# Attention output of batches two to eight from rounded parts and rests, three matmuls for one in fp32, with the units' steps moved

## The reference

```
q_s = exp(q - max_d q);  q_s = q_s / (sum_d q_s + 1e-9)
k_s = exp(k - max_s k);  k_s = k_s / (sum_s k_s + 1e-9)
kv  = k_s^T v                     (64 x 64 for each head)
attn = q_s kv                     -> x: 4608 tokens x 512
x = square(relu(x w_in)) w_out                               (512 -> 2048 -> 512)
x = rmsnorm(x) * rms_g;  out = (silu(x w_gate) * (x w_val)) w_out2   (512 -> 1536 -> 512)
```

## Time and profile before

| | us |
|---|---|
| median of 3 runs | 1733.18 |
| lowest and highest | 1731.26, 1733.26 |
| the profiled execution, whole | 1731.07 |
| its span from the first to the last instruction | 1729.3 |
| PE busy | 1697.3 (98%) |
| DVE, ACT, POOL busy | 1018.1, 567.7, 567.3 |
| mean granted TensorE clock | 0.997 |

### The profile page before, as it was taken

One profiled execution on the slowest core, in us unless ns is written; L12 is line 12 of the kernel. 1 busy time (PEld: TensorE's weight loads), 2 busy tenths in 40 slices (PEclk: granted clock), 3 DMA queues, 4 the chain that ended last, 5 costly groups with the idle time before them and its releaser, 6 DMA issues.

```text
span 1729.3 us, 23832 instructions
## 1 busy us (share of the span) xinstructions
PE 1697.3 (98%) x8954; PEld 1499.7 (87%) x8954; DVE 1018.1 (59%) x1525; ACT 567.7 (33%) x952; POOL 567.3 (33%) x442
## 2 busy tenths in 40 slices
PE   6999999999999999999999999999999999999999
PEld 5989999999988888888889898888899998888887
DVE  6667576667575778788776466446554455222220
ACT  5444333333232333333334333323333334212220
POOL 2554233323202224342255745546445521000000
PEclk9999999999999999999999999999999999999999
DMA  7575455445283353334342222242222245343341
GB/s 236 193 213 168 147 167 173 161 152 183 84 265 98 122 163 120 116 121 126 118 127 95 95 97 102 76 143 80 99 99 77 77 152 181 122 146 122 122 134 49
DMA packets 136722, 230.10 MB, mean 133 GB/s; under 512 B 12192, under 2 KB 59808, under 8 KB 136608
## 3 DMA queue, kind: packets, MB, share of 16 engines
q1 hardware_dynamic: 136608, 228.57, 40.6%
HBM read 143.59 MB, written 84.93 MB: 132 GB/s over the span
## 4 chain that ended last, share of the span: by engine, by line
PE 88%; DVE 5%; POOL 3%; issue 1%; ACT 1%; DMA 1%; SPq 0%; ACTq 0%; POOLq 0%; DVEq 0%
PE bank L1590 15%; PE bank L1592 14%; PE bank L1591 14%; PE bank L1676 7%; PE bank L1678 7%; PE bank L1677 7%; PE bank L1747 6%; PE bank L1748 6%; PE bank L1746 6%; PE bank L1564 2%; PE bank L1583 1%; DVE TAR L1296 1%; PE bank L1579 1%; POOL ssq L869 1%; DMA W<-in_w 0%
## 5 line engine op out<-in xcount | busy, mean ns | idle before, releaser
L1590 PE MATMUL bank<-TR,SW 128*128 128x460 f32 (+1 forms) x840 | 310.8, 370 | 2.2 <-ACT group L1142 1.8
L1591 PE MATMUL bank<-TR,SW 128*128 128x460 f32 (+1 forms) x840 | 310.1, 369 | 0.0
L1592 PE MATMUL bank<-TR,SW 128*128 128x460 f32 (+1 forms) x840 | 310.1, 369 | 0.0
L1590 PE MATMUL bank<-TAR,SA 128*128 128x288 f32 x784 | 247.8, 316 | 3.9 <-DVE TAR L1296 2.4
L1591 PE MATMUL bank<-TAR,SA 128*128 128x288 f32 x784 | 231.8, 296 | 0.0
L1592 PE MATMUL bank<-TAR,SA 128*128 128x288 f32 x784 | 231.2, 295 | 0.0
L1676 PE MATMUL bank<-GH,W 128*128 128x512 f32 x576 | 224.3, 389 | 0.7 <-DVE GH L1316 0.7
L1678 PE MATMUL bank<-GH,W 128*128 128x512 f32 x576 | 224.1, 389 | 0.0
L1677 PE MATMUL bank<-GH,W 128*128 128x512 f32 x576 | 224.1, 389 | 0.0
L1590 PEld LDWEIGHTS bank<-TR,SW 128*128 128x128 f32 x840 | 158.0, 188 | 21.9 <-issue 3.1
L1592 PEld LDWEIGHTS bank<-TR,SW 128*128 128x128 f32 x840 | 158.1, 188 | 16.7
(11 more groups left out here) (144 smaller groups left out, 2817.5 us busy)
## 6 DMA issues: line engine op xcount, KB each, us to landing
h_scratch<-hb SPq DMA_DIRECT2D x128, 288.0 KB, 2.7
hst<-h_scratch SPq DMA_DIRECT2D x144, 256.0 KB, 2.7
AR<-a_scratch SPq DMA_DIRECT2D x54, 512.0 KB, 3.7
a_scratch<-group SPq DMA_DIRECT2D x96, 230.0 KB, 2.0
xst<-xn_scratch SPq DMA_DIRECT2D x16, 920.0 KB, 5.0
xn_scratch<-x SPq DMA_DIRECT2D x9, 1024.0 KB, 5.3
out<-ost SPq DMA_DIRECT2D x36, 256.0 KB, 4.5
kt<-in_k SPq DMA_DIRECT2D x28, 320.0 KB, 4.5
```

Of the source, the lines that this page charges most:

```text
L1590: nc.tensor.matmul(ps[:, 0:w], w_hi[:, cc], x_hi[:, c], start=opens and c == 0, stop=False, skip_group_check=True)
L1591: nc.tensor.matmul(ps[:, 0:w], w_lo[:, cc], x_hi[:, c], start=False, stop=False, skip_group_check=True)
L1592: last = nc.tensor.matmul(ps[:, 0:w], w_hi[:, cc], x_lo[:, c], start=False, stop=c == 1, skip_group_check=True)
```

## The change

X0 and X1 of batches 1 to 7 become three fp32r matmuls. readQ0 and readQ1 on ACT now write the rounded part of qT (`qT` has two planes); two new DVE tasks `restQ0` and `restQ1` subtract that from the PSUM bank into the second plane. KV is read into `bd32`; a new ACT task `highKV` copies it, rounded, to `bdhi`, and a new DVE task `restKV` makes `bdlo`. A round that takes the bank of a Q round also waits for its rest (`q_rest`); X0 and X1 wait for `kv_rest` and `q_rest`. The tables move: the base of a unit is one step earlier, X0, X1 and their reads stay where they were, KM and KV come one step earlier, Q0 and Q1 with their reads two steps earlier, qmax, qsub, qexp, qsum, qinv and qnorm two steps earlier. A memory address (`STAT_END`) is fixed.

```diff
-UNIT_BASE = [[8 + 12 * c for c in range(KC)]] + [[6 + 11 * c for c in range(KC)]] * (B - 2)
-UNIT_PE = [("KM", -4), ("Q0", 0), ("Q1", 1), ("KV", 2), ("X0", 6), ("X1", 7)]
-UNIT_DVE = [("qmax", -10), ("qsum", -6), ("qinv", -6), ("kmax", -9), ("readKM", -3), ("readKV", 3)]
-UNIT_ACT = [("qexp", -7), ("kexp", -2), ("readQ0", 1), ("readQ1", 2), ("readX0", 7), ("readX1", 8)]
-UNIT_POOL = [("qsub", -9), ("qnorm", -4)]
+UNIT_BASE = [[7 + 12 * c for c in range(KC)]] + [[5 + 11 * c for c in range(KC)]] * (B - 2)
+UNIT_PE = [("KM", -4), ("Q0", -1), ("Q1", 0), ("KV", 2), ("X0", 7), ("X1", 8)]
+UNIT_DVE = [("qmax", -11), ("qsum", -7), ("qinv", -7), ("kmax", -9), ("readKM", -3), ("restQ0", 1), ("restQ1", 2),
+            ("readKV", 3), ("restKV", 5)]
+UNIT_ACT = [("qexp", -8), ("kexp", -2), ("readQ0", 0), ("readQ1", 1), ("highKV", 4), ("readX0", 8), ("readX1", 9)]
+UNIT_POOL = [("qsub", -10), ("qnorm", -5)]
 UNIT_SP = [("q", -20), ("kT", -19), ("kt", -17), ("v", -15)]
...
+        def rest_no(b, c, half):
+            return 2 * (unit(b, c) - KC - 1) + half + 1
...
                 wait_taken(eng, n - 2)
+                b, kind, c = ROUNDS[n - 2]
+                if kind[0] == "Q":
+                    eng.wait_ge(q_rest, rest_no(b, c, int(kind[1])))
...
+            def kv_hi(b, c):
+
+                wait_taken(act, ROUND_NO[b, "KV", c] - 1)
+                nc.scalar.activation(bdhi[:, :], bd32[:, :], ACT.Copy).then_inc(kv_high, 1)
...
+            def q_lo(b, c, half):
+
+                n = ROUND_NO[b, f"Q{half}", c]
+                cols = slice(0, Q_CUT * P) if half == 0 else slice(Q_CUT * P, S)
+                wait_taken(dve, n - 1)
+                nc.vector.tensor_tensor(qT[:, 1, cols], round_bank(n - 1)[:, 0:cols.stop - cols.start], f(qT[:, 0, cols]),
+                                        ALU.subtract).then_inc(q_rest, 1)
+
+            def kv_lo(b, c):
+
+                dve.wait_ge(kv_high, unit(b, c) - KC)
+                nc.vector.tensor_tensor(bdlo[:, :], bd32[:, :], f(bdhi[:, :]), ALU.subtract).then_inc(kv_rest, 1)
...
+                elif b:
+                    tok = slice(half * TA, (half + 1) * TA)
+                    pe.wait_ge(kv_rest, u - KC)
+                    pe.wait_ge(q_rest, rest_no(b, c, half))
+                    nc.tensor.matmul(ps[:, 0:TA], bdhi[:, :], qT[:, 0, tok], start=True, stop=False)
+                    nc.tensor.matmul(ps[:, 0:TA], bdlo[:, :], qT[:, 0, tok], start=False, stop=False)
+                    last = nc.tensor.matmul(ps[:, 0:TA], bdhi[:, :], qT[:, 1, tok], start=False, stop=True)
```

More of the change, by code:

```diff
@@ L25 @@
 NB4 = TB // P
+STAT_END = 211744
 EPS_RMS, EPS_SUM = 1e-6, 1e-9
@@ L300, in build @@
         ssqlo, at = place("ssqlo", at, [P, TB], F32R)
-        stat_end = at
+        assert at <= STAT_END
+        stat_end = at = STAT_END
         ones, at = place("ones", at, [P, P], F32R)
@@ L336, in build @@
         vn[1], at = place("vn1", at, [P, SJ, P + 1])
+        bd32, at = place("bd32", at, [P, P])
         assert at <= quad_at
@@ L342, in build @@
             kt[i], at = place(f"kt{i}", at, [P, SJ, P])
-        qT, at = place("qT", at, [P, S])
-        bd, at = place("bd", at, [P, P])
+        qT, at = place("qT", at, [P, 2, S], F32R)
+        bdlo, at = place("bdlo", at, [P, P], F32R)
+        bdhi, at = place("bdhi", at, [P, P], F32R)
         kmax, at = place("kmax", at, [P, 1])
@@ L386, in build @@
         q_sum, q_den, q_inv, q_norm = sem("q_sum"), sem("q_den"), sem("q_inv"), sem("q_norm")
+        q_rest, kv_high, kv_rest = sem("q_rest"), sem("kv_high"), sem("kv_rest")
         rnd_ready, taken_act, taken_dve = sem("rnd_ready"), sem("taken_act"), sem("taken_dve")
@@ L445, in bufs @@
             i = c % 2
-            return Bufs(kT[i][:, :], qn[i][:, :, :, :], vn[i][:, :, :], kt[i][:, :, :], qT[:, :], bd[:, :], kmax[:, :],
+            return Bufs(kT[i][:, :], qn[i][:, :, :, :], vn[i][:, :, :], kt[i][:, :, :], qT[:, :, :], bd32[:, :], kmax[:, :],
                         qmax[:, :, :])
@@ L787, in _ @@
                 lambda: nc.gpsimd.memset(vn[1][:, :, P:P + 1], 1.0),
-                lambda: nc.gpsimd.memset(bd[:, :], 0.0),
+                lambda: nc.gpsimd.memset(bd32[:, :], 0.0),
             ):
@@ L980, in take_round @@
                     cols = slice(0, Q_CUT * P) if half == 0 else slice(Q_CUT * P, S)
-                    nc.scalar.activation(m.qT[:, cols], ps[:, 0:cols.stop - cols.start], ACT.Copy).then_inc(taken_act, 1)
+                    qT_hi = m.qT[:, 0, cols] if b else m.qT[:, cols]
+                    nc.scalar.activation(qT_hi, ps[:, 0:cols.stop - cols.start], ACT.Copy).then_inc(taken_act, 1)
                 else:
@@ L1033, in task @@
                         take_round(what[4:], b, i)
+                elif what == "highKV":
+                    kv_hi(b, i)
                 elif what == "split":
@@ L1322, in task @@
                     take_round(what[4:], b, i)
+                elif what == "restKV":
+                    kv_lo(b, i)
+                elif what[:4] == "rest":
+                    q_lo(b, i, int(what[5:]))
                 elif what == "split":
```

## The result

The changed kernel takes 1777.75 us (median of 5 runs, 1776.27 to 1780.14) against 1733.18 (5 runs, 1731.26 to 1733.66): the ratio over all runs is 1.0264, 95% interval 1.0252 to 1.0275 (that of the two medians alone is 1.0257). It is slower by 45 us; the forecast was 32 slower, 1765, in a range of 1746 to 1782.

The account below looks back on a forecast made before the run. PE, busy for 98% of the span, was taken to bound the kernel. Five steady batches +27, batch 1's units +4 and batch 2's +2.5 make 33.5 on 1731.07: 1764.6, given as 1765, range 1746 to 1782.

Parts of the forecast that it names:

- X1 waits 0.96 after the step: Second and third unit: X1 waits for ACT's read of X0, 0.96 twice for 0.48 twice, adding 1.0 a batch.
- T4's hi ahead of readQ0: Turn of batches: ACT does T4's hi before readQ0, part of the chain making first KV wait 1.93; turn adds 2.0.
- restKV behind qsum: X0 waits for restKV, behind qnorm on POOL or qsum and qinv on DVE: 0.6, 0.55, 0.1 by unit.
- the clamp in step 0: Batch 1's units: negative steps fall into step 0, qsum and qinv precede kmax, KM waits 6 us in one piece.
- the prediction's own signs: Batch period 64.5 as forecast; near 62 means (1), near 66 with clock under 1 rival (2), under 59 wrong.
- rival (2): The clock falls at each turn of batches, five times 2.3 us more: 1777, chance 0.11.
- A steady batch: Units of batches 3 to 7: each batch +5.4 us (+3.0 without holding), five of them +27, low +15.
- Batch 2, forecast +2.5: Batch 2's units: waits of 2.2 at Q0 and 2.4 at KV, rest of the batch +2.9; +2.5 in all.
- Batch 1 was forecast at +4: Batch 1's units: +3.4 from the late kmax, +2.4 by the clock, less 1.0 at a KV and 0.7 for X.
- (4): X's three matmuls do not beat one fp32, gain 0: 1770; inside the forecast's 0.60 chance.
- (1): DVE and POOL get out of each other's way in the new order: about 1749, chance 0.19.
- (3): Faster: qnorm's earlier place on POOL decides, the loss at the turn to batch 1 goes: 1719, chance 0.06.

Follow-up runs that it names:

- the matmuls' run: Changed kernel with X as one fp32 matmul of the rounded parts, rests still made and waited for: 1781.91 us, ratio 1.0279.
- KM's run: Changed kernel with KM, readKM and kexp one step later: 1773.91 us, ratio 1.0237.
- T4's run: Changed kernel with the split of T4 two steps later on ACT and one on DVE: 1766.03 us, ratio 1.0197.
- its run: Changed kernel with restKV one step earlier, ahead of the next unit's qsum and qinv on DVE: 1769.37 us, ratio 1.0216.
- kmax's run: Changed kernel with kmax ahead of qsum and qinv on DVE in step 0: 1773.55 us, ratio 1.0236.
- The tables alone: Kernel before with the changed step tables only, X still one fp32 matmul and no rests: 1755.72 us, ratio 1.0128.
- W2's splits later: W2's splits three steps later on ACT and DVE: on the changed kernel 1780.29 us, ratio 1.0277; on the S-sums-later kernel 1732.04 us, 1.0001.
- the run with the S sums later: New arithmetic on the old tables, KM and X later, rests of Q earlier, plus group 4's S sums and splits seven steps later: 1732.93 us, ratio 1.0004.
- The best three: New arithmetic on old tables with KM later, rests of Q earlier: 1.0015; with X and S sums later too: 1.0004; with W2's splits later too: 1.0001.
- the steady batch of 58.7: From the kernel with the new arithmetic on the old tables, KM one step later and rests of Q one earlier: 1734.19 us, ratio 1.0015.

## Why the prediction was right, and where it was not

**The direction and the mechanism** held step by step: slower, in stage A alone, by the waits that were named. X gains 0.09 a round (the matmuls' run). X1 waits 0.96 after the step because KM took its place in the order of banks (KM's run). T4's hi ahead of readQ0 makes 1.0 of the first KV's wait (T4's run), restKV behind qsum those of X0 (its run), the clamp in step 0 some 4 us (kmax's run). The tables alone gave 22.7 where I had 25. By the prediction's own signs the batch period, 65.8, lies above the forecast's 64.5, near rival (2)'s 66, but at a clock of 1.00 (238 to 304 us), so not by that rival's cause.

**The size** was 32 for 45, so the sum was over a quarter short; that the time falls beside rival (2)'s 1777 is chance. By the trace, the missing 13 us (of 46.3 at the first matmul of stage B against 33.5):

- A steady batch grew by 6.66, not 5.4: over five batches 6.3. One wait I had not seen: the product behind KM at the turn (238.91, 0.53) waits for the bank that `h_12` of the batch before reads (T1 of a group waits for `h12_done` of the group two back), and `h_12` stood behind the held B21 split, 238.37 to 238.81. I had looked at T4's wait for `h_22`, 0.28, and not at the one ahead. Second, X0 of the second unit waited 0.90, not 0.55: restKV ended as forecast, 6.15 after KV's start, but PE started X0 0.26 after that end, where KV had started 0.10 after restQ0. Third, a wait also costs the step behind it about 0.1 (the matmul after the first starts 0.24 and not 0.13 later); I had priced none.
- The clock. Rival (2) came about in part: behind one of the five steady turns the granted clock was 0.50, the lower level, for 13 matmuls, 1.4 us. Half of that came back, since B22 then waited 0.36 in place of 1.12: that batch was 0.75 longer than its neighbours, where the rival had 2.3. In the other experiments that kept the 1.94 wait the clock fell behind none to four of the five; in the run that had none (W2's splits later) it fell twice elsewhere, behind X1's wait of 0.96 that follows one of 0.90 at X0. With the wait cut to 0.95 (T4's run) it fell nowhere in the steady batches. The Trainium skill ("TensorE: Matmul & The Clock Gate", "What's actually happening") ties the level to the array's recent activity; these rows agree in that each fall of the steady batches stands behind waits, and no turn was sure to fall or not to fall.
- Batch 2, forecast +2.5, grew by 6.1. The waits were 2.26 at Q0 (forecast 2.2) and 2.86 at KV (2.4). The lower clock held from 108.8 to 119.0, 3 us of it in KV's wait; before, it held to 112.2. I had set one against the other; it was longer. The forecast's own terms also come to more than its 2.5: 0.6 with a falling clock, and 3.4 (not 2.9) for the rest of the batch, 4.0.
- Batch 7's waits for `hb`: 5.2 for 1.7, 3.5 more in this trace than in that of before, which the sum put at nothing ("From stage B on nothing is touched" leaves batch 7's steps out). What sets them stays open, as said above.
- Batch 1 was forecast at +4 and was +2.5 where it joins batch 2 (KM at 103.5 for 101.8, a step earlier in the order). There I overstated the clock's share: 12 matmuls at 0.24, 1.3 us, not 2.4.

Those are 6.3 + 0.75 + 3.6 + 3.5 - 1.5 = 12.65, for the 12.8 looked for.

Two numbers of the prediction's working do not come out and change little: a batch before adds up to 57.6, not 57.5; and 1782, the range's upper end, takes all of (4), where half of it gives 1779.5. The measured time is below both.

**The rivals.** (1), no holds, is ruled out by the trace: restKV took 0.65 in the mean over 28 and 0.23 alone. (3) did not come, and the run with the S sums later shows how much of it was there: with them out of the way the turn to batch 1 gave a clock of 1.00, and 2.6 us in the medians where (3) counted on 4 + 2.3. (4) is ruled out by the matmuls' run: its steady batch grew by what X saves. (2) came once in five, above.

**What no run reached** is a kernel clearly faster than before. The best three are at 1.0001 to 1.0015. The gain of 4.9 us is used up by waits for the rests, which put some 1.2 us a unit on DVE, and in these traces by 2.8 to 3.9 us more of waits for `hb` in batch 7 than in the trace of before. The S sums later without the later X (on the steady batch of 58.7) was not run, and none of the four mends of the changed tables (KM, kmax, T4, restKV) was run together with another.

## What to carry to other kernels

Where a ring of two banks orders the rounds, moving one round by a step can change who shares a bank with whom: list the order of the rounds again, and ask of each what stands on the reader's engine ahead of the read. Before adding work to a second engine to make the first one's matmuls cheaper, price the longest chain at the busiest place, not the mean load (DVE was 59% busy both times), and look for every wait on that engine's results, the nearest first. A gain of 0.09 us a round is used up by a wait of half a microsecond at one round in six.

## What was not expected of the hardware

A store of 288 KB took 2.5 us in the middle. In the run with W2's splits later ACT waited up to 5.1 us for such a store while a load of 1 MB, issued just ahead of it on the same queue, was under way; from 515 us on these stores took 2.1 to 8.2 us, 6.2 in the middle. And after a wait of the same length, 1.94 us at the same place of a batch, the granted clock of the changed kernel fell in one batch and not in the other four, and in another run with the same wait (KM one step later) in four of five.
